# Attention, MoE and MLP on one core: scores negated and scaled in the matmul, and the exponential's bias and scale made by two independent operations

## The chip, the cores and the metric

One core of a Trainium2 chip. The metric is the device time of one execution in microseconds, from runs of the whole kernel. Engines: TensorE (PE; its weight loads are PEld), VectorE (DVE), ScalarE (ACT), GpSimd (POOL), SyncE (SP, here only DMA issues and waits).

## What is computed

Three stages in one launch. The change touches the first alone.

```python
q_bits = (einsum('bhsd,dk->bhsk', q, proj) > 0)          # 6 bits per token; k_bits likewise
mask   = q_bucket[:, :, :, None] == k_bucket[:, :, None, :]   # equal bits
scores = where(mask, q @ k.T / sqrt(D), -1e9)
scores = scores - max(scores, -1)
attn   = exp(scores);  attn /= sum(attn) + 1e-9
x      = attn @ v                                         # B=2, H=8, S=768, D=64
```

Then a top-1 mixture of 8 experts over 1536 tokens of width 512, and a dense MLP 512 to 2048 to 512 with an ELU.

## The kernel before

**Layout.** The 16 heads are taken in 8 pairs; a head has 6 units of 128 query rows, so 96 units. The loop over pairs is unrolled for the first and the last pair, and for a drain behind the last; the pairs between run in a hardware loop on each engine. Each engine has its program written out by hand, and counts on semaphores; nothing is scheduled by a planner. A *slot* is one step of that program: slot s of a pair works on unit s, and on older units at fixed lags. Below, slots are counted 0 to 5 within a head (u in the code, j is the head in the pair).

**How the mask enters.** A matmul has 128 rows to contract, and a head needs 64. Products are made from a high and a low part of each operand (fp32r), and spare rows carry the bucket bits. q and k are turned by TensorE (`turn_qk`), their high part is copied by ScalarE (`move_qk`, L772), the low part is the difference, taken by VectorE (`move_qk`, L922). `project` (L535 to L537) multiplies by proj, with signs, into 64 rows for q's bits and their complements and 64 for k's; VectorE's `move_bits` (L926) compares with a threshold `thr` and multiplies by `amp`, both one value per partition: 1 on the query's rows, -2^100 on the key's. SyncE's DMAs (`place_keys`, `place_bits`) put keys and bits in the halves where the scores matmuls want them. Each bit in which query and key differ adds -2^100 to the score.

**A slot, engine by engine.** In this order on each engine's own queue:

- TensorE: scores of unit n, four matmuls of 384 columns (L564, L565), when the exponential of unit n-2 has read the bank pair; in slots 0 and 1 `turn_qk` of the next head (L529), in slots 2 and 3 `project`; six transposes of unit n-2's probabilities (L581), each half of them when `pt_lo` of unit n-3 is done; in two slots of three the product with v (L593, L594); in slot 5 `finish_head` (L544). `turn_qk` shares a bank with `finish_head`, so in slot 0 it waits until VectorE has taken the finished rows (`prep_moved`).
- VectorE: the row maximum of the scores (L952, one reduction over 768 columns) into `stats`; then `move_qk` (slots 0, 1), `move_bits` (slots 2, 3), a reciprocal (slot 4, L959); the two `pt_lo` of unit n-2 (L965), behind ScalarE's copies; in slot 5 `move_rows` (L936, L938: logit_parts and x_rows).
- GpSimd: waits for the maximum; L432 makes the scale (max > -2^99) * 1/8; waits for that operation (`scale_ready`); L434 makes the bias -(max * scale). In slots 0 to 2 it also splits v and the first expert's weights, and behind the pair adds 1e-9 to the sums.
- ScalarE: `move_qk` in slots 0 and 1; two `pt_hi` copies of unit n-2 (L788); the exponential of unit n (L795) when bias and scale are ready, with both as values per partition and the row's sum accumulated; every third slot a copy of the product with v (L803).
- SyncE: loads of q, k, v and of the first expert's weights, `place_keys` and `place_bits`.

So where a row has no key in its bucket, the scale is 0 and the row is uniform. PSUM: `ps_s` four banks (two units), `ps_t` two, `ps_o` and `ps_p` one each; `ps_p` holds what the next head's preparation makes.

Lines outside the attention stage that the prediction uses for durations: L872 (a ScalarE copy with a scale per partition), L892 (an exponential without one), L1072 and L1127 (VectorE, 512 columns from PSUM: two tensors; one tensor and immediates).

Of the kernel before, what the change touches and what calls it, by code (L numbers as in the profile page):

```python
# [5 lines left out]
ALU = mybir.AluOpType  # L6
ACT = mybir.ActivationFunctionType
AX = mybir.AxisListType
# [12 lines left out]
def attention_moe_mlp(nc, q, k, v, proj, w_gate, w1, w2, w_in, w_out, out):  # L21
# [24 lines left out]
    NF = FF // P  # L46
    SCALE = float(D) ** -0.5
    BIG = 2.0 ** 100


    PROJ_SCALE = 2.0 ** 24
# [29 lines left out]
    with ExitStack() as ctx:  # L81
# [63 lines left out]
        probs, c = place("probs", [P, 4, S], F32, c)  # L145
        o_sb, c = place("o_sb", [P, S], F32, c)
        finish, c = place("finish", [P, H, XR], F32, c)
        stats, c = place("stats", [P, 3, 4], F32, c)
        sums, c = place("sums", [P, 2, QT], F32, c)
        inv, c = place("inv", [P, QT], F32, c)  # L150
        proj_sb, c = place("proj_sb", [P, NBITS], F32, c)
# [2 lines left out]
        nought, c = place("nought", [P, 1], F32, c)  # L154
        bits, c = place("bits", [P, S], F32R, c)
        thr, c = place("thr", [P, 1], F32, c)
        amp, c = place("amp", [P, 1], F32, c)
        logit_parts, c = place("logit_parts", [P, H, TT, E], F32, c)
        x_rows, c = place("x_rows", [P, TT, DM], F32, max(c, keep_end + 34 * 1024))

# [44 lines left out]
        def sem(name):  # L205
            return ctx.enter_context(nc.semaphore(name))
# [6 lines left out]
        keys_placed, placed = sem("keys_placed"), sem("placed")  # L213
        bits_made, gates_in, logits_moved = sem("bits_made"), sem("gates_in"), sem("logits_moved")
        split_v_hi, v_split = sem("split_v_hi"), sem("v_split")
        scale_ready, scored, max_found, bias_ready, exp_done = sem("scale_ready"), sem("scored"), sem("max_found"), sem("bias_ready"), sem("exp_done")
        guarded, inverted = sem("guarded"), sem("inverted")
        turned, hi_moved, lo_moved = sem("turned"), sem("hi_moved"), sem("lo_moved")
        weighted, o_moved, finished = sem("weighted"), sem("o_moved"), sem("finished")
# [163 lines left out]
        def _(pool):  # L383
# [39 lines left out]
            def body(i):  # L423
                for s in slots_of(i):
                    n = i * SPP + s
                    j, u = s // QT, s % QT
                    h = i * 2 + j
                    if live(i, s, 0, UNITS):
                        c = slice(s % 4, s % 4 + 1)
                        wait_apart(max_found, n + 1)  # L430

                        g.tensor_scalar(stats[:, 1, c], stats[:, 0, c], -BIG / 2, SCALE, ALU.is_gt, ALU.mult).then_inc(scale_ready, 1)  # L432
                        wait_apart(scale_ready, n + 1)
                        g.tensor_scalar(stats[:, 2, c], stats[:, 0, c], stats[:, 1, c], -1.0, ALU.mult, ALU.mult).then_inc(bias_ready, 1)  # L434
                        if u == 0:
                            split_v(j, h, 0)
                            split_weights(i, j, 0)
                        elif u == 1:
                            split_weights(i, j, 1)
                        elif u == 2:  # L440
                            split_v(j, h, 1)
                    if u == 2 and has_last(i, j):
                        wait_apart(exp_done, h * QT)
                        g.tensor_scalar(sums[:, 1 - j], sums[:, 1 - j], 1e-9, None, ALU.add).then_inc(guarded, 1)

            pairs(pool, body)


# [316 lines left out]
        def _(act):  # L765
# [3 lines left out]

            def move_qk(j, h, half, bank):  # L770
                act.wait_ge(qk_turned, h * 2 + half + 1)
                a(qk_hi[j][:, half * HW:(half + 1) * HW], bank[:, 0:HW], ACT.Copy).then_inc(qk_hi_moved, 1)  # L772

            def body(i):
                first = isinstance(i, int) and i == 0
                for s in slots_of(i):
                    n = i * SPP + s
                    j, u = s // QT, s % QT
                    h = i * 2 + j
                    if u in (0, 1) and has_next(i, j):  # L780
                        move_qk(1 - j, h + 1, u, ps_p)
                    if live(i, s, 2, UNITS):
                        gb, uu = (s - 2) // 3 % 2, (s - 2) % 3
                        if uu == 0 and not (first and s < 8):
                            act.wait_ge(weighted, i * 4 + (s - 2) // 3 - 1)
                        for half in range(2):
                            act.wait_ge(turned, n * 2 - 4 + half + 1)
                            a(pt_hi[gb][:, half * HALF:(half + 1) * HALF, uu * P:(uu + 1) * P],  # L788
                              ps_t[:, half, 0:HW].rearrange("p (t c) -> p t c", c=P), ACT.Copy).then_inc(hi_moved, 1)
                    if live(i, s, 0, UNITS):  # L790
                        c = slice(s % 4, s % 4 + 1)
                        act.wait_ge(bias_ready, n + 1)
                        if not (first and s < 4):
                            act.wait_ge(turned, n * 2 - 6)
                        a(probs[:, s % 4].rearrange("p (h c) -> p h c", h=2), ps_s[:, 2 * (s % 2):2 * (s % 2) + 2, 0:HW], ACT.Exp,  # L795
                          bias=stats[:, 2, c], scale=stats[:, 1, c], accum_out=sums[:, j, u:u + 1]).then_inc(exp_done, 1)
                    if live(i, s, 6, 2 * HEADS, 3) and (s - 6) % 3 == 0:
                        g = (s - 6) // 3
                        G = i * 4 + g
                        act.wait_ge(weighted, G + 1)  # L800
                        if g % 2 == 0 and not (first and g == 0):
                            act.wait_ge(finished, i * 2 + g // 2)
                        a(o_sb[:, g % 2 * HW:(g % 2 + 1) * HW], ps_o[:, 0:HW], ACT.Copy).then_inc(o_moved, 1)  # L803

            move_qk(0, 0, 0, ps_p)
            move_qk(0, 0, 1, ps_o)
            act.wait_ge(qk_hi_moved, 2)
# [108 lines left out]
        def _(dve):  # L916
            v_ = nc.vector

            def move_qk(j, h, half, bank):
                dve.wait_ge(qk_hi_moved, h * 2 + half + 1)  # L920
                cols = slice(half * HW, half * HW + HW)
                v_.tensor_tensor(qk_lo[j][:, cols], bank[:, 0:HW], qk_hi[j][:, cols].bitcast(F32), ALU.subtract).then_inc(prep_moved, 1)  # L922

            def move_bits(j, h, half, bank):
                dve.wait_ge(bits_made, h * 2 + half + 1)
                v_.tensor_scalar(bits[:, half * HW:(half + 1) * HW], bank[:, 0:HW], thr[:], amp[:], ALU.is_gt, ALU.mult).then_inc(prep_moved, 1)  # L926

            def move_rows(i, hf):
                dve.wait_ge(inverted, hf + 1)
# [11 lines left out]
            def body(i):  # L941
                if isinstance(i, int) and i == PAIRS:
                    dve.wait_ge(logits_moved, H)
                    add_logits(0)
                for s in slots_of(i):
                    n = i * SPP + s
                    j, u = s // QT, s % QT
                    h = i * 2 + j
                    if live(i, s, 0, UNITS):
                        c = slice(s % 4, s % 4 + 1)  # L950
                        dve.wait_ge(scored, n + 1)
                        v_.tensor_reduce(stats[:, 0, c], ps_s[:, 2 * (s % 2):2 * (s % 2) + 2, 0:HW], AX.XY, ALU.max).then_inc(max_found, 1)  # L952
                    if u in (0, 1) and has_next(i, j):
                        move_qk(1 - j, h + 1, u, ps_p)
                    if u in (2, 3) and has_next(i, j):
                        move_bits(1 - j, h + 1, u - 2, ps_p)
                    if u == 4 and has_last(i, j):
                        dve.wait_ge(guarded, h)
                        v_.reciprocal(inv[:], sums[:, 1 - j]).then_inc(inverted, 1)  # L959
                    if live(i, s, 2, UNITS):  # L960
                        gb, uu = (s - 2) // 3 % 2, (s - 2) % 3
                        for half in range(2):
                            dve.wait_ge(hi_moved, n * 2 - 4 + half + 1)
                            where = (slice(None), slice(half * HALF, (half + 1) * HALF), slice(uu * P, (uu + 1) * P))
                            v_.tensor_tensor(pt_lo[gb][where], ps_t[:, half, 0:HW].rearrange("p (t c) -> p t c", c=P),  # L965
                                             pt_hi[gb][where].bitcast(F32), ALU.subtract).then_inc(lo_moved, 1)
                    if u == FINISH_AT and has_last(i, j):
                        move_rows(i, h - 1)


            for q, (test, size) in enumerate(((ABOVE, 1.0), (NOT_ABOVE, 1.0), (NOT_ABOVE, -BIG), (ABOVE, -BIG))):
                v_.memset(thr[q * 32:q * 32 + 32, :], test)
                v_.memset(amp[q * 32:q * 32 + 32, :], size)
            v_.memset(proj_w[:].bitcast(F32), 0.0).then_inc(proj_split, 1)

            dve.wait_ge(const_in, 32)
# [4 lines left out]
            v_.tensor_tensor(proj_hl[:, 1], proj_sb[:], proj_hl[:, 0].bitcast(F32), ALU.subtract).then_inc(proj_split, 1)  # L981
            dve.wait_ge(proj_split, 4)
            for part in range(2):
                for q, sign in enumerate((1.0, -1.0, -1.0, 1.0)):
                    rows = slice(q // 2 * D, q // 2 * D + D)
                    v_.tensor_scalar(proj_w[rows, part, q * 32:q * 32 + NBITS], proj_hl[rows, part].bitcast(F32), sign, None, ALU.mult).then_inc(proj_ready, 1)
            move_qk(0, 0, 0, ps_p)
# [186 lines left out]
```

## Time and profile before

| | us |
|---|---|
| median of 3 runs (lowest, highest) | 862.69 (861.37, 862.85) |
| the profiled execution, its own time | 862.61 |
| its span, first to last instruction | 860.9 |
| TensorE busy in the span | 786.8 (91%) |
| VectorE, ScalarE, GpSimd busy | 400.8, 342.2, 380.9 |
| mean granted TensorE clock | 0.97 |

Attention ends at about 290 us, the experts take the stretch to about 580, the MLP the rest. Times in the rows are microseconds unless marked ns, counted from the span's start; L12 is line 12 of the kernel. Busy time of an engine overlaps that of the others. The chain of waits is followed back from the last instruction: at each step to what released it, or to the instruction before it on its engine. TensorE's matmuls are pipelined: a matmul of 384 columns whose weights were loaded in time is shown with 0.34 us but starts about 0.175 us behind the one before.

### The profile page before, as it was taken

What the parts mean: (1) busy time and instruction counts of PE and PEld (TensorE: products, weight loads), DVE (VectorE), ACT (ScalarE), POOL (GpSimd) and SP (SyncE); (2) the same over time, 40 slices, a digit from 0 to 9 for tenths busy, and PEclk for the clock granted to TensorE, in tenths of its full rate; (3) what the DMA queues carried; (4) which work ended last, traced back from release to release, by engine and by line L of the source; (5) the groups of instructions that cost most, each with busy time, mean ns of one, the idle gap of its engine ahead of it and who ended that gap; (6) DMA issues with size and microseconds to landing.
All of it is one profiled execution on the core that took longest, in us unless ns stands there. A gap on an engine that the chain in (4) does not pass through costs nothing.

```text
span 860.9 us, 13834 instructions
## 1 busy us (share of the span) xinstructions
PE 786.8 (91%) x4070; PEld 662.5 (77%) x4071; DVE 400.8 (47%) x696; ACT 342.2 (40%) x675; POOL 380.9 (44%) x462
## 2 busy tenths in 40 slices
PE   5899999999999319999999999959999999999998
PEld 4789988888888207888887778737888888888886
DVE  5888888887888501122212212213343443434333
ACT  5777777777778102122222122122232322222222
POOL 3334434433443179599999999149300000000000
PEclk9999999999999859999999999978999999999999
DMA  5556564454352065366566556224000100000001
GB/s 159 131 166 185 121 195 107 113 139 125 82 135 86 15 229 175 109 216 192 179 215 196 192 199 193 98 65 144 13 25 13 49 0 0 0 30 20 1 1 49
DMA packets 70732, 93.87 MB, mean 109 GB/s; under 512 B 32048, under 2 KB 34096, under 8 KB 70704
## 3 DMA queue, kind: packets, MB, share of 16 engines
q1 hardware_dynamic: 62528, 77.06, 30.6%
q10 hardware_dynamic: 6256, 10.16, 3.4%
q0 software_dynamic: 1920, 6.29, 2.2%
q8 instruction: 15, 0.25, 0.1%
q14 instruction: 13, 0.11, 0.0%
HBM read 59.54 MB, written 16.25 MB: 88 GB/s over the span
## 4 chain that ended last, share of the span: by engine, by line
PE 68%; issue 14%; POOL 6%; DMA 5%; DVE 4%; ACT 1%; SPq 1%; POOLq 1%; DVEq 0%
PE ps_s L628 9%; PE ps_s L630 9%; PE ps_s L629 9%; PE ps_t L581 6%; PE ps_t L726 5%; PE ps_t L728 5%; PE ps_t L727 5%; PE ps_o L593 4%; PE ps_o L594 4%; PE ps_s L564 3%; PE ps_s L565 3%; POOL w_lo L484 2%; POOL w_hi L480 2%; DMA late_stage<-in_moe_w_dram 2%; PE ps_p L544 2%
## 5 line engine op out<-in xcount | busy, mean ns | idle before, releaser
L795 ACT ACTIVATE probs<-ps_s,stats 128x768 f32<-128x768 f32 x96 | 95.3, 993 | 26.4 <-POOL stats L434 25.9
L965 DVE TENSOR_TENSOR pt_lo<-ps_t,pt_hi 128x384 fp32r<-128x384 f32 x192 | 97.0, 547 | 9.9 <-ACT pt_hi L788 9.6
L952 DVE TENSOR_REDUCE stats<-ps_s 128x1 f32<-128x768 f32 x96 | 91.5, 953 | 18.6 <-PE ps_s L565 18.3
L484 POOL TENSOR_TENSOR w_lo<-stage,w_hi 128x1024 fp32r<-128x1024 f32 x36 | 87.6, 2434 | 0.0
L581 PE MATMUL ps_t<-ident,probs 128*128 128x128 f32 x576 | 82.5, 277 | 5.1 <-DVE pt_lo L965 5.0
L484 POOL TENSOR_TENSOR w_lo<-late_stage,w_hi 128x1024 fp32r<-128x1024 f32 x36 | 86.9, 2435 | 0.0
L788 ACT ACTIVATE pt_hi<-ps_t 128x384 fp32r<-128x384 f32 x192 | 83.5, 490 | 7.8 <-PE ps_t L581 7.4
L432 POOL TENSOR_SCALAR stats<-stats 128x1 f32<-128x1 f32 x96 | 21.1, 220 | 145.7 <-DVE stats L952 145.6
L726 PE MATMUL ps_t<-yT_hi,w_hi 128*128 (+1 forms) x192 | 77.3, 402 | 2.2 <-DVE yT_lo L1110 1.4
L581 PEld LDWEIGHTS ps_t<-ident,probs 128*128 128x128 f32 x576 | 65.8, 140 | 16.4 <-DVE pt_lo L965 13.9
L727 PE MATMUL ps_t<-yT_lo,w_hi 128*128 (+1 forms) x192 | 76.8, 400 | 0.0
L728 PE MATMUL ps_t<-yT_hi,w_lo 128*128 (+1 forms) x192 | 76.7, 400 | 0.0
L628 PE MATMUL ps_s<-w_hi,gT_hi 128*128 128x512 f32 x192 | 76.6, 399 | 0.0
L629 PE MATMUL ps_s<-w_hi,gT_lo 128*128 128x512 f32 x192 | 75.9, 395 | 0.0
L630 PE MATMUL ps_s<-w_lo,gT_hi 128*128 128x512 f32 x192 | 75.8, 395 | 0.0
L892 ACT ACTIVATE elu_e<-elu_e 128x512 f32<-128x512 f32 x48 | 30.3, 632 | 112.3 <-DVE elu_e L1127 112.3
L564 PE MATMUL ps_s<-key_hi_hi,query_lo_hi 128*128 128x384 f32 x192 | 69.8, 364 | 4.4 <-DMA query_lo_hi<-query_hi_mask 2.3
L1078 DVE TENSOR_TENSOR hidT_lo<-ps_t,hidT_hi 128x512 fp32r<-128x512 f32 x38 | 26.1, 687 | 100.6 <-ACT hidT_hi L836 100.6
L593 PE MATMUL ps_o<-pt_hi,v_split 128*128 128x384 f32 x192 | 70.4, 367 | 1.2 <-DVE pt_lo L965 1.2
L628 PE MATMUL ps_s<-w_hi,xgT_hi 128*128 x152 | 62.8, 413 | 3.1 <-DVE xgT_lo L1072 1.7
L565 PE MATMUL ps_s<-key_lo_mask,query_hi_mask 128*128 128x384 f32 x192 | 65.2, 340 | 0.0
L594 PE MATMUL ps_o<-pt_lo,v_split 128*128 128x384 f32 x192 | 64.7, 337 | 0.0
(151 smaller groups left out, 1613.2 us busy)
## 6 DMA issues: line engine op xcount, KB each, us to landing
stage<-in_moe_w_dram SPq DMA_DIRECT2D x72, 256.0 KB, 3.0
late_stage<-in_moe_w_dram SPq DMA_DIRECT2D x56, 256.0 KB, 2.9
key_hi_hi<-query_hi_mask SPq DMA_DIRECT2D x30, 192.0 KB, 3.8
x_slots<-x_rows SPq DMA_DIRECT2D x19, 256.0 KB, 3.9
xg<-x_slots ACTq DMA_DIRECT2D x19, 256.0 KB, 3.1
y_slots<-y_sb ACTq DMA_DIRECT2D x19, 256.0 KB, 2.8
raw_qk<-in_q_dram SPq DMA_DIRECT2D x16, 192.0 KB, 3.2
raw_v<-in_v_dram SPq DMA_DIRECT2D x16, 192.0 KB, 2.6
```

The costliest lines, as they stand in the source:

```text
L484: g.tensor_tensor(wl[:, ds(at + c * CH, CH)], stages[c % 4].rearrange("p m f -> p (m f)"), wh[:, ds(at + c * CH, CH)].bitcast(F32), ALU.su ...
L564: mm(to, qk_lo[j][:, u * P:(u + 1) * P], key_hi[j][:, cols], start=True, stop=False)
L581: last = nc.tensor.transpose(ps_t[:, half, t * P:(t + 1) * P], probs[:, (s - 2) % 4, kt * P:(kt + 1) * P], ident[:])
L593: mm(ps_o[:, 0:HW], v2[jv][:, kt].rearrange("p a d -> p (a d)"), pt_hi[gb][:, kt], start=kt == 0, stop=False)
L594: last = mm(ps_o[:, 0:HW], v2[jv][:, kt].rearrange("p a d -> p (a d)"), pt_lo[gb][:, kt], start=False, stop=kt == QT - 1)
L628: mm(to, x_hi, wh[:, w], start=start, stop=False)
L629: mm(to, x_lo, wh[:, w], start=False, stop=False)
L630: return mm(to, x_hi, wl[:, w], start=False, stop=stop)
L726: mm(ps_t[:, f % 2], wa, ya, start=k == 0, stop=False)
L727: mm(ps_t[:, f % 2], wa, yb, start=False, stop=False)
L728: last = mm(ps_t[:, f % 2], wb, ya, start=False, stop=k == KD - 1)
L965: v_.tensor_tensor(pt_lo[gb][where], ps_t[:, half, 0:HW].rearrange("p (t c) -> p t c", c=P), pt_hi[gb][where].bitcast(F32), ALU.subtract). ...
```

## The change

TensorE now gives the negative of the scaled score: q's high and low parts are multiplied by -1/8 when they leave PSUM (the k rows by 1), by a value per partition `side`, on ScalarE and VectorE; proj's rows for q are divided by it again. Bits are 0 or 2^50 on both sides, so that a differing bit adds 2^100. The row statistic is the minimum. GpSimd makes bias = (min < 2^99) * min and scale = (min < 2^99) * -1, both from the minimum, with no wait between them; `scale_ready` is gone, `bias_ready` counts two per unit. `stats` is laid out by slot. GpSimd waits for its five setup operations before the loop, ScalarE for VectorE's memsets before its first copy.

```diff
+    HALF_BIG = 2.0 ** 50
...
-        stats, c = place("stats", [P, 3, 4], F32, c)
+        stats, c = place("stats", [P, 4, 4], F32, c)
...
-        amp, c = place("amp", [P, 1], F32, c)
+        side, c = place("side", [P, 1], F32, c)
...
@@ GpSimd, body
-                        c = slice(s % 4, s % 4 + 1)
-                        wait_apart(max_found, n + 1)
-
-                        g.tensor_scalar(stats[:, 1, c], stats[:, 0, c], -BIG / 2, SCALE, ALU.is_gt, ALU.mult).then_inc(scale_ready, 1)
-                        wait_apart(scale_ready, n + 1)
-                        g.tensor_scalar(stats[:, 2, c], stats[:, 0, c], stats[:, 1, c], -1.0, ALU.mult, ALU.mult).then_inc(bias_ready, 1)
+                        c = s % 4
+                        wait_apart(least_found, n + 1)
+                        g.tensor_scalar(stats[:, c, 2:3], stats[:, c, 0:1], BIG / 2, stats[:, c, 0:1], ALU.is_lt, ALU.mult).then_inc(bias_ready, 1)
+                        g.tensor_scalar(stats[:, c, 3:4], stats[:, c, 0:1], BIG / 2, -1.0, ALU.is_lt, ALU.mult).then_inc(bias_ready, 1)
...
+            pool.wait_ge(made, 5)
             pairs(pool, body)
...
@@ ScalarE
-                a(qk_hi[j][:, half * HW:(half + 1) * HW], bank[:, 0:HW], ACT.Copy).then_inc(qk_hi_moved, 1)
+                a(qk_hi[j][:, half * HW:(half + 1) * HW], bank[:, 0:HW], ACT.Copy, scale=side[:]).then_inc(qk_hi_moved, 1)
...
-                        act.wait_ge(bias_ready, n + 1)
+                        act.wait_ge(bias_ready, n * 2 + 2)
...
-                          bias=stats[:, 2, c], scale=stats[:, 1, c], accum_out=sums[:, j, u:u + 1]).then_inc(exp_done, 1)
+                          bias=stats[:, c, 2:3], scale=stats[:, c, 3:4], accum_out=sums[:, j, u:u + 1]).then_inc(exp_done, 1)
...
+            act.wait_ge(proj_split, 1)
             move_qk(0, 0, 0, ps_p)
...
@@ VectorE
-                v_.tensor_tensor(qk_lo[j][:, cols], bank[:, 0:HW], qk_hi[j][:, cols].bitcast(F32), ALU.subtract).then_inc(prep_moved, 1)
+                v_.scalar_tensor_tensor(qk_lo[j][:, cols], bank[:, 0:HW], side[:], qk_hi[j][:, cols].bitcast(F32), ALU.mult, ALU.subtract).then_inc(prep_moved, 1)
...
-                v_.tensor_scalar(bits[:, half * HW:(half + 1) * HW], bank[:, 0:HW], thr[:], amp[:], ALU.is_gt, ALU.mult).then_inc(prep_moved, 1)
+                v_.tensor_scalar(bits[:, half * HW:(half + 1) * HW], bank[:, 0:HW], thr[:], HALF_BIG, ALU.is_gt, ALU.mult).then_inc(prep_moved, 1)
...
-                        v_.tensor_reduce(stats[:, 0, c], ps_s[:, 2 * (s % 2):2 * (s % 2) + 2, 0:HW], AX.XY, ALU.max).then_inc(max_found, 1)
+                        v_.tensor_reduce(stats[:, c, 0:1], ps_s[:, 2 * (s % 2):2 * (s % 2) + 2, 0:HW], AX.XY, ALU.min).then_inc(least_found, 1)
...
-            for q, (test, size) in enumerate(((ABOVE, 1.0), (NOT_ABOVE, 1.0), (NOT_ABOVE, -BIG), (ABOVE, -BIG))):
+            for q, test in enumerate((ABOVE, NOT_ABOVE, NOT_ABOVE, ABOVE)):
                 v_.memset(thr[q * 32:q * 32 + 32, :], test)
-                v_.memset(amp[q * 32:q * 32 + 32, :], size)
+            v_.memset(side[0:D, :], -SCALE)
+            v_.memset(side[D:P, :], 1.0)
...
-                for q, sign in enumerate((1.0, -1.0, -1.0, 1.0)):
+                for q, sign in enumerate((-1.0 / SCALE, 1.0 / SCALE, -1.0, 1.0)):
```

## Rows read from the trace of the kernel before

**Rows 1.** Page, part 2: TensorE's busy tenths in 40 equal slices of the span.

```profile
PE   5899999999999319999999999959999999999998
```

**Rows 2.** Waits from 20 to 290 us: waiter, releaser, us in total, times, longest.

```profile
ACT probs L795 <- POOL stats L434: 24.6, 60, 0.7
...
POOL stats L434 <- POOL stats L432: 14.8, 72, 0.2
PEld ps_t L581 <- DVE pt_lo L965: 13.9, 37, 1.0
...
PEld ps_p L535 <- DVE query_lo_hi L922: 1.1, 7, 0.2
```

**Rows 3.** Chain of waits, 150 to 175 us: start us, us, what.

```profile
159.10 0.53 DVE pt_lo L965
...
163.88 0.57 DVE x_rows L938
...
164.50 0.55 PE ps_p L529 x3
```

**Rows 4.** Timeline, slots 0 and 1: start us, us, engine, line, operation, [idle <-releaser].

```profile
165.08 0.49 ACT L772 ACTIVATE query_hi_mask<-ps_p 128x384 fp32r<-128x384 f32 x1 [2.06 <-PE ps_p L529]
...
165.60 0.56 DVE L922 TENSOR_TENSOR query_lo_hi<-ps_p,query_hi_mask 128x384 fp32r<-128x384 f32 x1 [0.30 <-ACT query_hi_mask L772]
...
167.49 0.96 DVE L952 TENSOR_REDUCE stats<-ps_s 128x1 f32<-128x768 f32 x1 [0.40 <-PE ps_s L565]
...
167.82 0.49 ACT L772 ACTIVATE query_hi_mask<-ps_p 128x384 fp32r<-128x384 f32 x1
...
168.37 0.55 DVE L922 TENSOR_TENSOR query_lo_hi<-ps_p,query_hi_mask 128x384 fp32r<-128x384 f32 x1
...
168.81 0.34 PE L565 MATMUL ps_s<-key_lo_mask,query_hi_mask 128*128 128x384 f32 x1
...
168.97 0.19 PEld L535 LDWEIGHTS ps_p<-query_hi_mask,proj_w 128*128 128x128 f32 x1
168.99 0.43 PE L535 MATMUL ps_p<-query_hi_mask,proj_w 128*128 128x384 f32 x1
```

**Rows 5.** Timeline of TensorE: first and last of the late projection matmuls.

```profile
33.62 0.43 PE L535 MATMUL ps_p<-query_hi_mask,proj_w 128*128 128x384 f32 x1
...
253.86 0.42 PE L535 MATMUL ps_p<-query_hi_mask,proj_w 128*128 128x384 f32 x1
```

**Rows 6.** Groups by line and shape, whole span: count, busy us, mean ns, idle before.

```profile
L1127 DVE TENSOR_SCALAR elu_e<-ps_t 128x512 f32<-128x512 f32 x48 | 33.0, 688 | 47.3 <-PE ps_t L728 47.3
...
L926 DVE TENSOR_SCALAR bits<-ps_p,thr,amp 128x384 fp32r<-128x384 f32 x30 | 20.1, 670 | 0.0
L922 DVE TENSOR_TENSOR query_lo_hi<-ps_p,query_hi_mask 128x384 fp32r<-128x384 f32 x31 | 17.1, 553 | 4.4 <-ACT query_hi_mask L772 4.3
L1072 DVE TENSOR_TENSOR xgT_lo<-ps_o,xgT_hi 128x512 fp32r<-128x512 f32 x19 | 13.1, 692 | 34.3 <-ACT xgT_hi L828 34.3
...
L892 ACT ACTIVATE elu_e<-elu_e 128x512 f32<-128x512 f32 x48 | 30.3, 632 | 112.3 <-DVE elu_e L1127 112.3
...
L872 ACT ACTIVATE yg<-yg,gate 128x512 f32<-128x512 f32 x12 | 8.6, 719 | 14.0 <-DMA yg<-y_slots,pos 13.9
...
L434 POOL TENSOR_SCALAR stats<-stats 128x1 f32<-128x1 f32 x96 | 25.4, 265 | 17.2 <-POOL stats L432 14.8
```

**Rows 7.** Timeline of GpSimd: the pair's second operation and the one behind it.

```profile
171.33 0.27 POOL L434 TENSOR_SCALAR stats<-stats 128x1 f32<-128x1 f32 x1 [0.21 <-POOL stats L432]
...
171.56 1.02 POOL L411 TENSOR_TENSOR v_split<-raw_v,v_split 128x384 fp32r<-128x384 f32 x1
```

**Rows 8.** Chain of waits in the last pair of heads.

```profile
266.80 0.21 POOL stats L432
...
267.11 0.28 POOL stats L434
```

**Rows 9.** Chain of waits, first 30 us.

```profile
6.99 1.03 DVE query_lo_hi L922 x2
```

More of the change, by code:

```diff
@@ L215, in attention_moe_mlp @@
         split_v_hi, v_split = sem("split_v_hi"), sem("v_split")
-        scale_ready, scored, max_found, bias_ready, exp_done = sem("scale_ready"), sem("scored"), sem("max_found"), sem("bias_ready"), sem("exp_done")
+        scored, least_found, bias_ready, exp_done = sem("scored"), sem("least_found"), sem("bias_ready"), sem("exp_done")
         guarded, inverted = sem("guarded"), sem("inverted")
@@ L790, in body @@
                     if live(i, s, 0, UNITS):
-                        c = slice(s % 4, s % 4 + 1)
-                        act.wait_ge(bias_ready, n + 1)
+                        c = s % 4
+                        act.wait_ge(bias_ready, n * 2 + 2)
                         if not (first and s < 4):
@@ L949, in body @@
                     if live(i, s, 0, UNITS):
-                        c = slice(s % 4, s % 4 + 1)
+                        c = s % 4
                         dve.wait_ge(scored, n + 1)
-                        v_.tensor_reduce(stats[:, 0, c], ps_s[:, 2 * (s % 2):2 * (s % 2) + 2, 0:HW], AX.XY, ALU.max).then_inc(max_found, 1)
+                        v_.tensor_reduce(stats[:, c, 0:1], ps_s[:, 2 * (s % 2):2 * (s % 2) + 2, 0:HW], AX.XY, ALU.min).then_inc(least_found, 1)
                     if u in (0, 1) and has_next(i, j):
```

## The prediction

> **What bounds the kernel now.** I read the page's busy slices first: TensorE is nine tenths busy through attention, which runs from the first slices to the dip after slice 13 [rows 1]. Everything the change touches lies in that stage, so I price that stage alone. A busy row does not say which wait ends last, so I then read the waits of that stretch. The pair of GpSimd operations that the change reworks looks promising there: ScalarE waited 24.6 us in 60 places for it, and inside the pair the second operation waited 14.8 us for the first [rows 2]. But TensorE itself waited for VectorE: its weight loads lost 13.9 us to pt_lo, the low halves of the transposed probabilities [rows 2]. So I read the chain of waits, which alone decides. It repeats with every head, and a head takes about 17 us. It is TensorE work but for two short pieces of VectorE: in slot 4 the row reduction and, behind it, pt_lo (159.10 us), and at the end of a head x_rows (163.88 us), for which the next transposes start at 164.50 us [rows 3]. The same two pieces stand there head after head, and up to the last pair of heads the chain passes neither the GpSimd pair nor the exponential. That is the first conclusion: the wait which the change removes belongs to an engine with slack.
>
> The second comes from the timeline of slot 1 of one head, where the next head's q and k are split [rows 4]. TensorE transposes them, ScalarE copies the high part (L772, 167.82 us, 0.49), VectorE subtracts (L922, 168.37 us, 0.55, so to 168.92), and TensorE loads the weights of the projection at 168.97 us. TensorE had started its last scores matmul at 168.81 and would have loaded at once behind it: the load is late by about 0.15, and the first projection matmul shows 0.43 where a prefetched one shows 0.34 [rows 4]. So L772 and L922 are on TensorE's path already, with no slack left. The first and the last such late matmul are at 33.62 and 253.86 us, and there are 14, one per head [rows 5]. The chain prints this only as a long first matmul, and the wait is small in the table (1.1 us, 7 times) [rows 2], but it has no cushion.
>
> **The change part by part.**
>
> *GpSimd pair.* Today: 0.21 for L432 [rows 8], 0.21 of gap [rows 7], then L434 at 0.265 [rows 6]. Two operations that do not wait start closer: behind L434 the next operation starts 0.23 later (171.33 to 171.56) [rows 7]. So the bias pair ends about 0.20 earlier in the loop. ScalarE gets its exponential sooner, and spends that waiting for TensorE's transposes. Cover: TensorE's own work and the two VectorE pieces. Without cover it would be 0.20 per unit. It counts only in the last pair of heads, where no preparation of another head fills TensorE: the chain passes the pair there twice, with 0.31 between the starts (266.80, 267.11) [rows 8]. Twice (0.31 - 0.23) is 0.16, and with a second operation of 0.22 to 0.265 about **-0.2 us**. Bounds: 0, and -0.5 if a few more units of that pair join.
>
> *ScalarE copy L772 gets a pointer scale.* The trace has no PSUM copy with a pointer scale. The nearest rows are the copy with a pointer scale (L872, 719 ns) and an activation of the same 128x512 between the same memories without one (L892, 632 ns): 87 ns [rows 6]. The copy with a pointer (L872) shows it although its engine had waited before it, and ScalarE waits for TensorE before L772 too, so nothing hides the 87 ns. Of them, part goes into slack: VectorE is free for L922 about 0.88 after the reduction's start at 167.49, so at 168.37, while ScalarE's result was ready at 168.31. Where VectorE does wait for it, in slot 0, it starts 0.03 behind ScalarE's end (165.57 to 165.60) [rows 4], so here it could have started at 168.34. So L922 starts later by 0.087 - 0.03 = 0.057. Bounds 0 and 0.087.
> The Trainium skill ("ScalarE: Activation LUTs", section on what ACT_TABLE_LOAD costs) says that every per-partition pointer operand adds about 93 ns to an ACTIVATE; it speaks against this change, and with it the sum would end 0.1 us higher.
>
> *VectorE L922 becomes scalar_tensor_tensor with a pointer scalar.* Two pointers cost in L926: 670 ns at 128x384, against 688 at 128x512 without any (L1127). Two tensors at both widths (692, 553) give 139 for the 128 columns, so L1127 at 384 would be about 549 to 555, and two pointers cost 115 to 121, one about 58 [rows 6]. Bounds: 0, and 120 if the first pointer carries the whole price; I take 58, since ScalarE's price per pointer is of that order and the form itself has no reason to be dearer.
>
> *Together on the path.* The projection's weights come 0.057 + 0.058 = 0.115 us later, in 14 heads: **+1.6 us** [rows 4 to 6]. I find nothing that takes it back: both VectorE pieces on the chain start from a TensorE result (scores of slot 4, end of the head), and shift whole. Slot 0 has the same copies but TensorE does not wait for them there. In the setup two L922 of 1.03 us stand on the chain (6.99 us) [rows 9], so 2 x 0.058 = **+0.1**. The second head's copies are covered, because the DMA of its keys lands after them.
>
> *L926 loses a pointer*: 0.06 less in slots 2 and 3, where VectorE is early anyway; TensorE waits for bits nowhere in rows 2. Zero; if it mattered it would be a gain of 28 x 0.06 = 1.7.
>
> *Minimum for maximum*: same tile, one pass, 0.96 [rows 4]; zero. The trace has no minimum; a nanosecond more would count once per head. *Powers, signs and the immediates of proj_w*: same instructions, zero. *Fewer memsets* at VectorE's start, before it waits for a DMA: zero. *New waits*: ScalarE waits for those memsets before its first copy, which waits for the first q and k anyway, GpSimd for its own copies ended long before unit 0; zero. The bias wait counts twice as far, with a multiply on ScalarE's queue, ahead of an exponential with slack.
>
> Sum: +1.6 + 0.1 - 0.2 = **+1.5 us** on the profiled execution's 862.61, so 864.1. Its time is 0.08 under the median of 862.69, which is nothing. The measurement tells about 0.2%, that is 1.7 us, from no change, so 864.1 counts as within it, barely.
>
> **Rivals.**
>
> *Dear pointer (slower).* The first pointer on VectorE carries all of the 120 ns. Place: slot 1, L922. Then each head loses 0.057 + 0.12 = 0.177: 14 x 0.177 + 0.24 - 0.2 = +2.5, **865.1**. It turns the result to slower from 0.13 per head on. For it: no row has one pointer. Against: ScalarE's single pointer shows a price of its own.
>
> *The slack was not slack (faster).* If the earlier exponential moves ScalarE's pt_hi and VectorE's pt_lo in slot 4 as well, TensorE's stall there shrinks by up to 0.20 per head, 16 x 0.2 = -3.2, and if VectorE is what holds slots 2 and 3, the cheaper L926 gives its 1.7 too: 862.61 - 3.2 - 1.7 + 1.7 = **859.4**. For: 24.6 us of ScalarE idle. Against: in slot 4 pt_lo starts right behind VectorE's own reduction and reciprocal, not behind ScalarE.
>
> *ScalarE's delay disappears.* If VectorE could not take L922 before the reduction has wholly ended (168.45), the 87 ns would be covered: 14 x 0.058 + 0.1 - 0.2 = +0.7, **863.3**. Against: L922 starts at 168.37, before 168.45 [rows 4].
> This is what the Trainium skill ("VectorE: DVE Perf Modes", section on the DRAIN) describes, the next instruction held until the pipe is empty; the row contradicts it.
>
> *The change does not do what it says*: the two operations do not overlap. Then only the -0.2 is missing: 864.3.
>
> **How the numbers follow.** Forecast with its pointer terms near 0.115, the missing overlap included: 0.71; its own spread of about 1 us puts 0.25 of that above 864.4. Dear pointer 0.15, faster 0.07, delay gone 0.07. So slower is 0.25 + 0.15 = 0.40, same 0.46 + 0.07 = 0.53, faster 0.07. The range runs from 862.4, pointers nearly free, to 866.0, dear pointer and a little of the run's spread (1.5 us between the three runs of before); it leaves out the faster case.
>
> **What would show it.** Right: L772 near 0.58 and L922 near 0.61, L926 near 0.61; the projection's weight load about 0.11 later behind the last scores matmul in 14 heads; the pair's starts 0.23 apart; a head longer by 0.11; the chain still free of GpSimd up to the last pair; MoE and MLP unchanged. Wrong: a head shorter than before, L922 unchanged at 0.55, or the late weight load grown by 0.2. A reduction longer than 0.96 would break the sum in another place.

## The result, and the profile after

The changed kernel takes 865.78 us (median of 5 runs, 864.09 to 867.60) against 862.69 (861.14 to 862.85): 1.0043 of before, 95% interval 1.0032 to 1.0055. The forecast was 864.1, within 0.2%, and the time lies inside the stated range; but the kernel is clearly slower, which had 0.40, and the change is +3.1 us where +1.5 was added up, about twice as much. The profiled execution took 865.78 us with a span of 864.1, so 3.2 us more span than before. Run again later beside other kernels, the same kernel came to 865.57 against 862.76, 1.0028 (1.0014 to 1.0042). The five runs of the result spread over 3.5 us against 1.7 of before; later, 12 runs of it spread over 4.2 us and 29 of before over 4.3. The last section shows where some of that comes from. The ratios leave out one execution, of before_swap_o, that took 1137.5 us at a mean granted clock of 0.65.

The page of the changed kernel, parts 1 and 2:

```profile
span 864.1 us, 13762 instructions
...
PE   5899999999999409999999999958999999999998
```

TensorE's row looks like [rows 1]; the page shows nothing of the cause. The groups by line and shape show the prices (count, busy us, mean ns, idle before):

```profile
L927 DVE TENSOR_SCALAR bits<-ps_p,thr 128x384 fp32r<-128x384 f32 x30 | 18.3, 609 | 0.0
...
L923 DVE SCALAR_TENSOR_TENSOR query_lo_hi<-ps_p,side,query_hi_mask 128x384 fp32r<-128x384 f32 x31 | 19.2, 618 | 6.9 <-ACT query_hi_mask L772 6.9
...
L772 ACT ACTIVATE query_hi_mask<-ps_p,side 128x384 fp32r<-128x384 f32 x31 | 18.0, 582 | 31.7 <-PE ps_p L529 31.2
...
L432 POOL TENSOR_SCALAR stats<-stats 128x1 f32<-128x1 f32 x96 | 28.8, 300 | 151.4 <-DVE stats L953 151.2
L433 POOL TENSOR_SCALAR stats<-stats 128x1 f32<-128x1 f32 x96 | 20.6, 215 | 7.6
```

The names moved a line or so: L923 is the former L922, L927 the former L926, L433 the former L434. Against [rows 4] and [rows 6]: ScalarE's copy 582 ns for 491 (0.49 in [rows 4]), VectorE's low part 618 for 553, the bits 609 for 670. A *pointer* here is an operand that the engine reads as one value per partition. So one pointer costs ScalarE 91 ns and VectorE 61 in the bits, where nothing else changed in form, and 65 in the low part, where the instruction changed its form too. GpSimd's first operation compares as the former one did, but now multiplies by a value per partition instead of a constant, and takes 300 ns where the former took 220.

The timeline of slot 1 in one head of the changed kernel, to be laid beside [rows 4]:

```profile
169.53 0.96 DVE L953 TENSOR_REDUCE stats<-ps_s 128x1 f32<-128x768 f32 x1 [0.24 <-PE ps_s L565]
...
169.86 0.58 ACT L772 ACTIVATE query_hi_mask<-ps_p,side 128x384 fp32r<-128x384 f32 x1
...
170.47 0.62 DVE L923 SCALAR_TENSOR_TENSOR query_lo_hi<-ps_p,side,query_hi_mask 128x384 fp32r<-128x384 f32 x1
...
170.70 0.30 POOL L432 TENSOR_SCALAR stats<-stats 128x1 f32<-128x1 f32 x1 [0.96 <-DVE stats L953]
...
170.84 0.34 PE L565 MATMUL ps_s<-key_lo_mask,query_hi_mask 128*128 128x384 f32 x1
...
171.08 0.21 POOL L433 TENSOR_SCALAR stats<-stats 128x1 f32<-128x1 f32 x1
171.14 0.19 PEld L535 LDWEIGHTS ps_p<-query_hi_mask,proj_w 128*128 128x128 f32 x1 [0.29 <-DVE query_lo_hi L923]
...
171.43 0.34 PE L536 MATMUL ps_p<-query_hi_mask,proj_w 128*128 128x384 f32 x1
```

From the last scores matmul (170.84) to the second projection matmul (171.43) it is 0.59 us; before it was 168.81 to 169.25, 0.44. Three rows of before for this place, beside those of [rows 4]:

```profile
168.65 0.23 POOL L432 TENSOR_SCALAR stats<-stats 128x1 f32<-128x1 f32 x1 [0.86 <-DVE stats L952]
...
169.08 0.26 POOL L434 TENSOR_SCALAR stats<-stats 128x1 f32<-128x1 f32 x1 [0.21 <-POOL stats L432]
...
169.25 0.34 PE L536 MATMUL ps_p<-query_hi_mask,proj_w 128*128 128x384 f32 x1
```

TensorE now waits for VectorE by 0.29, in all 14 heads, as the waits from 20 to 290 us say:

```profile
ACT probs L795 <- POOL stats L433: 21.7, 48, 0.7
...
PEld ps_t L581 <- DVE pt_lo L966: 13.9, 38, 0.9
...
PEld ps_p L535 <- DVE query_lo_hi L923: 4.1, 14, 0.3
```

Before, the last of these was 1.1 us in 7 places [rows 2]. The wait of ScalarE for the GpSimd pair fell from 24.6 us to 21.7, and nothing on the chain noticed. The pair of GpSimd operations now runs from 170.70 to 171.29, 0.59 where it was 0.69 (168.65 to 169.34). What that does to a pair of heads is read from the start of the first transposes of q and k, TensorE's timeline. First the kernel before, then the changed one:

```profile
130.54 0.55 PE L529 MATMUL ps_p<-ident,raw_qk 128*128 128x128 f32 x3 [0.71 <-DVE x_rows L938]
```

```profile
132.31 0.55 PE L529 MATMUL ps_p<-ident,raw_qk 128*128 128x128 f32 x3 [0.71 <-DVE x_rows L939]
...
166.54 0.55 PE L529 MATMUL ps_p<-ident,raw_qk 128*128 128x128 f32 x3 [0.71 <-DVE x_rows L939]
```

Before, the next but one head started at 164.50 [rows 3]: 33.96 us for two heads. After it is 34.23. That is 0.27 more per pair of heads, 0.135 per head, the same within 0.02 us in every pair of the loop.

So attention lengthens by about 1.9 us through 14 heads. But the span grew by 3.2. The rest is at the start, in the chain of the first 12 us of the changed kernel:

```profile
4.85 0.89 PE ps_p L529 x3
...
5.75 0.02 ACTq L771
...
5.80 1.28 ACT L772
...
7.10 0.59 ACT query_hi_mask L772
...
7.71 1.15 DVE query_lo_hi L923 x2
```

The third row has no counterpart in the prediction. L772 at 5.80 us for 1.28 us is ScalarE's load of its activation table. In the kernel before it ran at 1.53 us, under the first DMA. Now it stands behind the wait for the turned q and k (the ACTq row), and the first copy starts at 7.10 where it started at 5.88. The first scores matmul came at 13.11 instead of 12.30. The rows of before:

```profile
1.53 1.28 ACT L772 ACT_TABLE_LOAD   x1 [1.53 <-PEq L1161]
...
5.88 0.49 ACT L772 ACTIVATE query_hi_mask<-ps_p 128x384 fp32r<-128x384 f32 x1 [3.06 <-PE ps_p L529]
...
12.30 0.66 PE L564 MATMUL ps_s<-key_hi_hi,query_lo_hi 128*128 128x384 f32 x1 [1.89 <-ACT query_hi_mask L815]
```

and the first scores matmul of the changed kernel:

```profile
13.11 0.66 PE L564 MATMUL ps_s<-key_hi_hi,query_lo_hi 128*128 128x384 f32 x1 [1.85 <-ACT query_hi_mask L816]
```

### The profile page after: what moved, and what is told of

It reads as the page before. It is cut to its first block, busy times and chain, and to the rows that moved or that the text cites. A ratio compares the mean times of both kernels' runs of the same rounds, so it can differ in the third digit from the quotient of the medians.

```text
span 864.1 us, 13762 instructions
## 1 busy us (share of the span) xinstructions
PE 788.5 (91%) x4070; PEld 662.8 (77%) x4071; DVE 401.9 (47%) x694; ACT 344.2 (40%) x675; POOL 385.2 (45%) x462
## 4 chain that ended last, share of the span: by engine, by line
PE 68%; issue 13%; POOL 6%; DMA 6%; DVE 4%; ACT 1%; SPq 1%; POOLq 1%; DVEq 1%; ACTq 0%
PE ps_s L628 9%; PE ps_s L630 9%; PE ps_s L629 9%; PE ps_t L581 6%; PE ps_t L726 5%; PE ps_t L728 5%; PE ps_t L727 5%; PE ps_o L593 4%; PE ps_o L594 3%; POOL w_lo L484 3%; PE ps_s L564 3%; PE ps_s L565 3%; DMA late_stage<-in_moe_w_dram 2%; POOL w_hi L480 2%; PE ps_p L529 2%
## 5 line engine op out<-in xcount | busy, mean ns | idle before, releaser
L432 POOL TENSOR_SCALAR stats<-stats 128x1 f32<-128x1 f32 x96 | 28.8, 300 | 151.4 <-DVE stats L953 151.2
L581 PEld LDWEIGHTS ps_t<-ident,probs 128*128 128x128 f32 x576 | 65.8, 140 | 16.2 <-DVE pt_lo L966 13.9
```

The costliest lines, as they stand in the source:

```text
L581: last = nc.tensor.transpose(ps_t[:, half, t * P:(t + 1) * P], probs[:, (s - 2) % 4, kt * P:(kt + 1) * P], ident[:])
```

## The experiments

All periods below are of two heads in the loop, read as above from one profiled execution each; all ratios are to the kernel before, run beside it, with 95% intervals. "First scores" is the start of the first scores matmul.

**table_early.** The changed kernel with a tiny copy ahead of ScalarE's waits.

```diff
+            act.wait_ge(made, 2)
+            a(warm[:], nought[:], ACT.Copy)      # 128x1
```

> The changed kernel with one addition: ScalarE copies a single column (128x1) as soon as GpSimd's first memsets are there, before its waits for proj_split and for the turned q and k. Theory A (the span grew at the start because the activation table, 1.28 us, is now loaded behind the wait for the first turned q and k, at 5.80 us, where before it was loaded at 1.53 us): the table load moves back under the first DMA, the first scores matmul comes about 0.7 to 0.85 us earlier than in the changed kernel (13.11), and the whole kernel is faster than the changed one by about that: 1.002 to 1.003 of before. Rival B (the late start is chance, from the landing of the first DMAs): the table load moves but the first scores matmul stays near 13.1 on average and the time stays at 1.004.

Its timeline:

```profile
1.53 1.28 ACT L771 ACT_TABLE_LOAD   x1 [1.53 <-PEq L1166]
...
2.83 0.20 ACT L771 ACTIVATE warm<-nought 128x1 f32<-128x1 f32 x1
...
5.76 0.58 ACT L775 ACTIVATE query_hi_mask<-ps_p,side 128x384 fp32r<-128x384 f32 x1 [2.74 <-DVE proj_hl L984]
```

The load is back at 1.53 us, first scores at 12.43 (changed: 13.11), span 863.0, two heads still 34.23. Ratio 1.0025 (1.0012 to 1.0039), which alone does not tell it from the changed kernel. Theory A holds for the start. The last row names proj_hl as what the copy waited for, since it is the latest event on that semaphore; the wait asks only for its first count, VectorE's memset of proj_w, which ended at about 1.8 us.

**before_wait.** The kernel before, and on ScalarE one line more.

```diff
+            act.wait_ge(proj_split, 1)
             move_qk(0, 0, 0, ps_p)
```

> The kernel before with one addition: ScalarE's wait for proj_split ahead of its first copy, the wait that the change adds, and nothing else. Theory A (this wait is what puts the table load behind the wait for q and k): table load at about 5.8 us, first scores matmul 0.7 to 0.8 us later than the 12.30 of before, time about +0.8 us (1.001). Rival C (the pointer operand of the first copy is what moves it): table load stays at 1.5 us, time unchanged.

The chain of its first 14 us:

```profile
5.85 0.02 ACTq L771
...
5.91 1.28 ACT L772
```

and the first scores matmul in its timeline:

```profile
13.04 0.66 PE L564 MATMUL ps_s<-key_hi_hi,query_lo_hi 128*128 128x384 f32 x1 [1.89 <-ACT query_hi_mask L816]
```

The same picture as in the changed kernel, without any pointer: the added wait alone puts the table load behind the wait for the turned q and k, and first scores go from 12.30 to 13.04. Rival C falls. Two heads take 33.96 as before, and the span is 0.7 us longer (861.6 against 860.9). The time's ratio, 1.0003 (0.9992 to 1.0014), can't tell 0.7 us from none; the trace can: with the load at 1.53 us first scores lie between 12.04 and 12.43 in ten profiles, with the load behind the wait between 13.04 and 13.29 in three. table_early_again, changed_again and the reordered kernels below are among them.

**no_pointers, no_act_pointer, no_dve_pointer.** table_early with one or both pointers removed.

```diff
-            a(qk_hi[j][...], bank[:, 0:HW], ACT.Copy, scale=side[:])
+            a(qk_hi[j][...], bank[:, 0:HW], ACT.Copy)                       # not in no_dve_pointer
-            v_.scalar_tensor_tensor(qk_lo[j][...], bank[:, 0:HW], side[:], qk_hi[j][...], ALU.mult, ALU.subtract)
+            v_.tensor_tensor(qk_lo[j][...], bank[:, 0:HW], qk_hi[j][...], ALU.subtract)   # not in no_act_pointer
```

> table_early with both pointers taken away: ScalarE's copy of q and k without the scale, VectorE's low part as a plain subtraction of two tensors. This leaves out the scaling and the sign of q, so the exponentials are of other numbers; the instructions and their sizes are the same. The GpSimd pair and the cheaper bits operation stay. Theory A (the two pointers on the path of slot 1 are the whole loss per head): a pair of heads back at 33.96 us from 34.23, the copy at 0.49 and the subtraction at 0.55, time within 0.5 us of before, 0.9995 to 1.000. Rival D (part of the loss per head is the GpSimd pair, whose first operation now takes 0.30 us, or the doubled count that ScalarE waits for): a pair of heads stays above 34.05 and the time at 1.001 or more.

> table_early without the scale of ScalarE's copy of q and k; VectorE's pointer stays. This leaves out the scaling of the high parts. Theory A (ScalarE's 0.09 us counts less 0.03 of slack, VectorE's 0.065 counts whole): a pair of heads at 33.96 + 2 x 0.07 = 34.10 us, between the 33.96 without pointers and the 34.23 with both. Rival F (only one of the two matters, the other hides behind it): 34.23 or 33.96.

> table_early with ScalarE's scale kept and VectorE's low part as a plain subtraction of two tensors, 0.55 us. This leaves out the scaling in the low parts. Theory A: a pair of heads at 33.96 + 2 x 0.06 = 34.08 us; the excess of this run over 33.96 and of no_act_pointer over 33.96 add up to the 0.27 of both. Rival F: 34.23 or 33.96.

The groups from 20 to 290 us, first of no_act_pointer, then of no_dve_pointer:

```profile
L926 DVE SCALAR_TENSOR_TENSOR query_lo_hi<-ps_p,side,query_hi_mask 128x384 fp32r<-128x384 f32 x28 | 17.1, 612 | 3.9 <-ACT query_hi_mask L775 3.9
...
L775 ACT ACTIVATE query_hi_mask<-ps_p 128x384 fp32r<-128x384 f32 x28 | 13.8, 491 | 30.7 <-PE ps_p L530 29.2
```

```profile
L775 ACT ACTIVATE query_hi_mask<-ps_p,side 128x384 fp32r<-128x384 f32 x28 | 16.3, 582 | 28.7 <-PE ps_p L530 28.3
...
L926 DVE TENSOR_TENSOR query_lo_hi<-ps_p,query_hi_mask 128x384 fp32r<-128x384 f32 x28 | 15.6, 558 | 4.8 <-ACT query_hi_mask L775 4.8
```

| | copy, ns | low part, ns | two heads, us | over 33.96, per head |
|---|---|---|---|---|
| no_pointers | 491 | 552 | 33.95 | 0.00 |
| no_act_pointer (VectorE's stays) | 491 | 612 | 34.07 | 0.055 |
| no_dve_pointer (ScalarE's stays) | 582 | 558 | 34.11 | 0.075 |
| both (table_early) | 582 | 618 | 34.23 | 0.135 |

The parts add up (0.055 + 0.075 = 0.13) and rival F falls: each pointer counts by itself. The pairs of heads within a run differ by up to 0.04 us, and one pair of no_dve_pointer took 34.30, so the parts are good to about 0.01 per head. no_pointers, which keeps the GpSimd pair, its slower first operation, the doubled count and the cheaper bits, is level with before: 0.9993 (0.9981 to 1.0004), two heads 33.95. So rival D falls too, and with it any worth of the pair: what the change was about moved the time by nothing that could be seen, in either direction (the interval leaves room for 1.6 us of gain).

**changed_again, table_early_again.** Both once more, on one chip.

> The changed kernel once more, on the same chip as the next run. Theory A: first scores matmul at about 13.1 us again, table load at about 5.8; 0.8 us slower than table_early on the same chip. Rival B: the start moves by chance, and first scores matmul and time fall within 0.3 us of table_early.

> table_early once more, beside changed_again. Theory A: first scores matmul at about 12.4 us, a pair of heads at 34.23 us as in changed_again, time about 0.8 us under it. Rival B: within 0.3 us.

First scores 13.29 and 12.23, two heads 34.23 in both, medians 865.57 and 864.55: 1.0 us apart, which is what theory A has, but with 12 runs each that spread over 4 us it is not clear of none. The ratios, 1.0028 (1.0014 to 1.0042) and 1.0023 (1.0010 to 1.0036), overlap. So the time does not show the table load, and its size rests on the traces' 0.7 to 1.1 us at first scores. The two profiled spans, 865.6 and 861.3, are further apart than the start explains; 1.5 us of it is the slower end of attention that the last section shows.

**before_swap, before_swap3.** The chain of [rows 3] shows a larger stall than any the change touched: TensorE waits for x_rows before it turns the next q. In before_swap the six transposes of the probabilities go first, on TensorE alone; in before_swap3 ScalarE and VectorE follow the same order.

```diff
@@ TensorE, slot 0
-                    turn_qk(0)          # waits for x_rows
                     transposes of unit n-2
+                    turn_qk(0)
@@ ScalarE, slot 0 (before_swap3 only)
-                    move_qk(...)
                     pt_hi x2
+                    move_qk(...)
@@ VectorE, slot 0 (before_swap3 only)
-                    move_qk(...)
                     pt_lo x2
+                    move_qk(...)
```

> The kernel before with one reordering on TensorE: in slot 0 of a head the six transposes of the probabilities go ahead of the first half of the transposes of the next head's q and k, which wait for VectorE's x_rows. Theory A (the stall of 0.5 to 0.7 us for x_rows is on TensorE's path in every head and nothing else ends there): the transposes (0.66 us) fill it, a pair of heads shrinks by 2 x 0.5 to 0.66 us, and the time falls by 7 to 10 us, 0.988 to 0.992. Rival E (VectorE, which does about 14.9 us of work in a head of 17, ends the wait next): the stall moves to the waits for pt_lo or for the low part of q and k, and less than 3 us is gained.

> The kernel before with the order of slot 0 changed on three engines: TensorE does the probabilities' transposes ahead of those of the next q and k, ScalarE its two pt_hi copies ahead of its copy of q and k, VectorE its two pt_lo ahead of the low part of q and k. Theory (in before_swap ScalarE and VectorE still took q and k first, so pt_hi and pt_lo of slot 0 waited for the later transposes and pushed the low part of slot 1, for which TensorE's projection now waited 8.5 us instead of 1.1): the projection's wait goes back to 1 to 3 us, a pair of heads falls from 33.60 to 33.0 or below, time 5 to 8 us under before (0.991 to 0.994). Rival E (VectorE's own work in slots 0 and 1, about 5.0 us against 4.4 of TensorE, is the limit in whatever order): the pair stays at 33.5 to 33.7, time as before_swap, 0.997 to 0.999.

The wait for x_rows from 20 to 290 us in the kernel before:

```profile
PEld ps_p L529 <- DVE x_rows L938: 10.5, 12, 1.0
```

The waits of the same stretch, before_swap first, then before_swap3:

```profile
PEld ps_p L535 <- DVE query_lo_hi L924: 8.5, 14, 0.6
...
PEld ps_p L529 <- DVE x_rows L940: 2.6, 11, 0.3
```

```profile
PEld ps_t L579 <- DVE pt_lo L969: 13.9, 37, 1.0
...
PEld ps_p L535 <- DVE query_lo_hi L926: 5.2, 12, 0.4
...
PEld ps_p L529 <- DVE query_lo_hi L926: 2.9, 11, 0.3
PEld ps_p L529 <- DVE x_rows L942: 2.3, 10, 0.3
```

Two heads fall from 33.96 to 33.60 in the one and 33.59 in the other, not to 33.0. Filling the wait for x_rows (10.5 us before, 2.6 after) moved it to the low part of q and k. In before_swap3 that knot loosened (8.5 to 5.2 us), and a new wait for the same tile came up at the next transposes (2.9 us). Time: 0.9987 (0.9974 to 0.9999) and 0.9972 (0.9961 to 0.9982), median 859.84 against 862.13. The second is the version that beats both kernels, by 2.3 us over before. My theory of the order explains the knot and not the period; rival E has the period.

**changed_swap3.** table_early with the same three reorderings.

> table_early with the same new order of slot 0 on three engines. If the knot of slot 1 is where the pointers cost, and the new order leaves it on the path: 0.27 us more per pair of heads than before_swap3, about 1.9 us in all. If the new order gives slot 1 slack: the difference between the two shrinks below 0.1 per pair and the changed kernel is level with before_swap3.

Two heads take 33.75, so 0.16 more than before_swap3: between the two forecasts of 0.27 and under 0.1. Ratio 0.9982 (0.9967 to 0.9996). The pointers still cost, but less; I read that as other work of VectorE now also ending the wait, which is not shown.

**before_swap_o.** before_swap3 with ScalarE's copy of the product with v, at a head's start, moved behind the copy of q and k.

```diff
@@ ScalarE
-   slot 0: ..., exponential, copy of the product with v
-   slot 1: move_qk, pt_hi x2, ...
+   slot 0: ..., exponential
+   slot 1: move_qk, copy of the product with v, pt_hi x2, ...
```

> before_swap3 with ScalarE's copy of the product with v moved, at the head's start, from the end of slot 0 to behind its copy of q and k in slot 1. Theory (in slot 1 VectorE waits 0.37 us for ScalarE's copy of q and k, which stands behind that other copy, and TensorE's projection waits for VectorE): the copy of q and k starts about 0.3 us sooner, the low part too, the projection's wait shrinks, and a pair of heads falls from 33.59 to 33.1 to 33.3; time 0.995 to 0.996 of before. Rival E (VectorE's work of slots 0 to 2 is the limit): 33.5 or more, time as before_swap3, 0.997.

```profile
PEld ps_t L579 <- DVE pt_lo L975: 20.3, 66, 1.0
...
PEld ps_p L529 <- DVE query_lo_hi L932: 3.2, 12, 0.3
...
PEld ps_p L535 <- DVE query_lo_hi L932: 0.3, 2, 0.2
```

The projection's wait is gone (5.2 us to 0.3), and the wait for pt_lo has grown from 13.9 to 20.3 us, in 66 places instead of 37. Two heads take 33.57. Three orders in slots 0 and 1, three places for the wait, one period. I read that as VectorE's own sequence of work being the limit there. It is not shown: making that work shorter was not tried, and VectorE still waits for ScalarE within slots 0 and 1, 0.37 us for the copy of q and k in before_swap3 and 0.21 us for pt_hi in before_swap_o. Time 0.9988 (0.9973 to 1.0003), no better than before_swap3; its profile also has 1.8 us of slower clock at attention's end (last section), so the periods compare the two orders, the times do not.

## Why the prediction was wrong, and where it was right

**The step that failed** is the one under "New waits": "ScalarE waits for those memsets before its first copy, which waits for the first q and k anyway, GpSimd for its own copies ended long before unit 0; zero." The wait itself is indeed over long before, at about 1.8 us. But it changed what stands in front of what: with one wait before the first activation the table load ran ahead of it, with two it runs behind, and 1.28 us of load went onto the path. The start had 0.5 us of cover for it: ScalarE's first copy came 1.22 later (5.88 to 7.10), VectorE's low part only 0.72 (6.99 to 7.71), because before VectorE had its own proj_w to finish until 6.96. So a term that was put at zero measured +0.7. before_wait shows it alone (+0.74 at first scores), table_early undoes it. I had asked when the wait ends, and not what is queued behind it. The trace of before shows the load at 1.53 us, and I had left it out of my rows.
The Trainium skill ("ScalarE: Activation LUTs", its step-by-step section on what each stage is for) says that the compiler places the table load right before the activation that needs it. The rows agree: it is ScalarE's last instruction ahead of its first activation, in the one kernel ahead of that activation's wait, in the other behind it. The section on what ACT_TABLE_LOAD costs gives the load about 1283 ns, and the rows have 1.28 us.

**Right: where the change costs.** The chain passes none of the GpSimd pair in the loop, the wait that was removed had slack, and the knot is slot 1: copy, low part, projection, in 14 heads. The four durations came as forecast: 582 (0.58), 618 (0.61), 609 (0.61), and the minimum at 954 ns (the maximum 953).

**Right mechanism, size a little off: "0.057 + 0.058 = 0.115 us later, in 14 heads: +1.6 us".** Measured 0.135 per head, 1.9 us. VectorE's part was right (0.055 alone). ScalarE's part was 0.075 alone rather than 0.057. The slack that I subtracted was there: in slot 1 the low part starts 0.55 behind the start of the copy in the kernel before (167.82 to 168.37) and 0.61 in the changed one (169.86 to 170.47), 0.06 later for a copy that takes 0.09 longer, and VectorE now starts 0.03 behind the copy's end, as in slot 0. A pointer of 91 ns instead of 87 gives a few thousandths more; the rest of the difference, about 0.01 per head, is of the size that the pairs of heads differ by.

**Wrong in size: the pair.** "So the bias pair ends about 0.20 earlier" came out as 0.10, since the first operation takes 300 ns and not 220, and the second starts 0.38 behind the first, not 0.23. I had taken the spacing from the operation behind L434 and given the new first operation none of its own. The -0.2 at the end of attention did not come: from the last turning of q and k to the first scatter of rows it is 45.93 us before and 46.10 after. The last pair of heads is written out and not in the loop, and there the old pair was already closer together: 0.31 between the starts and 0.59 in all (266.80 to 267.39) [rows 8]. The chain of the changed kernel has it at 0.60:

```profile
269.69 0.30 POOL stats L432
...
270.07 0.22 POOL stats L433
```

What the shorter spacing in the loop gave (0.42 to 0.38) was off the path, and in the last pair of heads, where the pair is on it, the slower first operation ate all of it.

**Right: "+0.1" in the setup.** The two low parts on the chain take 1.15 us where they took 1.03 [rows 9].

The sum with the measured terms, against the span: start +0.8 (the table load 0.7, the two low parts 0.1), 14 heads +1.9, the end of attention 0, together 2.7; the first scatter comes 2.9 later (301.01 against 298.10) and the end 3.2 later. The last few tenths I can't place; they are smaller than the differences between executions. Against the forecast's +1.5, the table load makes 0.7 of what was missing, the size in the loop 0.3 and the gain at the end that did not come 0.2.

**Rivals.** The dear pointer (865.1) had nearly the time and the wrong reason: the first pointer on VectorE costs 61 to 65 ns, not 120. "Slack was not slack" and "ScalarE's delay disappears" are refuted by no_pointers and no_dve_pointer. Against the latter the prediction says that a row contradicts the section on the DRAIN in the Trainium skill ("VectorE: DVE Perf Modes"); that section goes on to say that an instruction which is not held starts earlier, so the row at 168.37 agrees with the whole of it. That the pair does not overlap was true: the second operation starts 0.08 behind the end of the first, and the time is none the worse for it.

## What to carry to other kernels

When a wait is removed from an engine, read whether the chain passes it; when an operation on the path gets a per-partition operand, price the operand, because 60 to 90 ns on a knot without slack is paid once per pass, whatever the wait elsewhere saves. Before adding a wait ahead of ScalarE's first activation, look where the table load runs in the trace, and if it ends up behind the wait, give the engine a tiny activation first. And where two engines are nearly full, moving a stall shows the next one at once: TensorE's 0.7 us for x_rows was worth 0.18 per head, not 0.7.

## What the runs showed of the hardware that I had not expected

ScalarE's table load ran at 1.53 or 1.54 us in every kernel with one wait before the first activation, and behind the waits, at 5.80, 5.91 and 5.98, in the three profiles with two. Whether the number of waits decides it or something else about them was not tried.

GpSimd takes 300 ns for a 128x1 comparison with a constant and multiplication by a value per partition, 265 for a multiplication by a value per partition and one by a constant, and 215 to 220 for a comparison and a multiplication with constants alone. So one pointer costs it 45 to 85 ns, by the form; why was not tried. Two dependent operations with a semaphore between them start mostly 0.41 to 0.44 us apart in the loop and 0.31 to 0.33 where the pairs of heads are written out; that too was not followed up.

A piece of the spread between executions sits at the end of attention. In changed_again the last products with v of attention ran at the lower of TensorE's two clocks: the granted clock is 1.00 up to 286 us, 0.93 from 286 to 288 and 0.50 (1.2 GHz) from 288 to 290, where the profile of the changed kernel has 1.00 throughout. The rows, first of changed_again, then of the changed kernel:

```profile
288.56 0.52 PE L594 MATMUL ps_o<-pt_lo,v_split 128*128 128x384 f32 x1
...
292.14 1.53 PE L544 MATMUL ps_p<-finish,o_sb 128*128 128x72 f32 x12 [0.67 <-ACT o_sb L803]
```

```profile
289.10 0.34 PE L594 MATMUL ps_o<-pt_lo,v_split 128*128 128x384 f32 x1
...
290.46 1.53 PE L544 MATMUL ps_p<-finish,o_sb 128*128 128x72 f32 x12 [0.67 <-ACT o_sb L803]
```

A matmul of 384 columns takes 0.52 us there instead of 0.34, and finish_head starts 1.7 us later though the last turning of q and k was only 0.15 later. Ahead of the fall TensorE had run at 2.4 GHz through pauses: from 286 to 288 us it was busy for 0.83 us, in both profiles alike. no_act_pointer, no_dve_pointer, changed_swap3 and before_swap_o show it too: 47.3 to 47.8 us from last turning to scatter, against 45.9 to 46.3 in the eight profiles without it. So it is not a matter of one kernel; whether a later or longer attention makes it likelier stays open.
